# Seven block products in place of eight for the experts' first products, from group 5 on

## The reference, cut to what matters

```python
# attention with 32 packed rows per head; then, on x [2304, 512] (4 batches of 576 tokens):
def _moe_ref(x, w_gate, w1, w2):            # w1 [8, 512, 1024], w2 [8, 1024, 512]
    P = ...                                 # gates [2304, 8], 8 rounds of row and column scaling
    for e in range(8):
        h = np.maximum(x @ w1[e], 0.0)
        out += P[:, e:e + 1] * (h @ w2[e])
# then a two-layer MLP on the result (w_in [512, 2048], w_out [2048, 512])
```

## Time and profile before

| | |
|---|---|
| median of three runs | 1747.98 us |
| the profiled execution's own time | 1750.12 us |
| its span, first to last instruction | 1748.3 us |
| granted TensorE clock | 0.998 of full |
| PE busy | 1740.7 us (100%) |
| DVE / ACT / POOL busy | 909.5 / 709.8 / 608.7 us |
| mean DMA rate | 45 GB/s |

### The profile page before, as it was taken

The page is one execution under the profiler, slowest core; times in us unless marked ns, Lnnn a source line. Parts: engine busy times, 40 slices in busy tenths (PEclk is TensorE's granted clock), DMA queues, the critical chain, the costliest instruction groups (busy, mean ns, idle before and its releaser), DMA issues.

```text
span 1748.3 us, 27319 instructions
## 1 busy us (share of the span) xinstructions
PE 1740.7 (100%) x10257; PEld 1517.9 (87%) x10257; DVE 909.5 (52%) x1363; ACT 709.8 (41%) x1564; POOL 608.7 (35%) x380
## 2 busy tenths in 40 slices
PE   9999999999999999999999999999999999999999
PEld 7888888898889888988889888988888888888887
DVE  4846645444554454445444544454546555555545
ACT  4644465444434443444344443444343222222222
POOL 1254334444444344444444344444441001111100
PEclk9999999999999999999999999999999999999999
DMA  8431111111211111111211111112000000000002
GB/s 263 125 85 40 47 37 37 37 37 37 59 36 38 46 36 36 36 36 48 48 36 48 36 36 36 36 36 59 25 25 24 13 25 25 25 24 24 0 0 108
DMA packets 71776, 78.81 MB, mean 45 GB/s; under 512 B 7984, under 2 KB 59184, under 8 KB 71728
## 3 DMA queue, kind: packets, MB, share of 16 engines
q1 hardware_dynamic: 71728, 78.15, 16.6%
HBM read 73.42 MB, written 4.72 MB: 45 GB/s over the span
## 4 chain that ended last, share of the span: by engine, by line
PE 99%; ACT 0%; DMA 0%; SPq 0%; DVE 0%; issue 0%
PE PS L1223 96%; PE PS L1243 2%; PE PS L1457 0%; DMA k_raw<-k_dram 0%; ACT g_raw L621 0%; ACT acc L651 0%; PE PS L1427 0%; ACT acc L621 0%; SPq L441 0%; DVE stat L894 0%; DVE acc L1019 0%; SPq L422 0%; SPq L417 0%; ACT a_parts L621 0%; DVE stat L895 0%
## 5 line engine op out<-in xcount | busy, mean ns | idle before, releaser
L1223 PE MATMUL PS<-w_hi,h_hi 128*128 128x512 f32 x1440 | 562.9, 391 | 0.0
L1223 PE MATMUL PS<-w_hi,h_lo 128*128 128x512 f32 x1440 | 560.9, 390 | 0.0
L1223 PE MATMUL PS<-w_lo,h_hi 128*128 128x512 f32 x1440 | 560.7, 389 | 0.0
L1024 DVE SCALAR_TENSOR_TENSOR acc<-PS,gate,acc 128x512 f32<-128x512 f32 x504 | 378.0, 750 | 267.0 <-PE PS L1223 267.0
L698 ACT ACTIVATE h_hi<-PS 128x576 fp32r<-128x576 f32 x256 | 167.0, 653 | 671.6 <-PE PS L1223 670.9
L1223 PE MATMUL PS<-a_parts,g_parts 128*128 128x288 f32 x3072 | 438.2, 295 | 0.0
L1223 PEld LDWEIGHTS PS<-a_parts,g_parts 128*128 128x128 f32 x3072 | 419.4, 188 | 5.3 <-issue 0.4
L621 ACT ACTIVATE g_raw<-PS 32x256 f32<-32x256 f32 x992 | 372.8, 376 | 14.6 <-PE PS L1223 0.6
L1005 DVE SCALAR_TENSOR_TENSOR h_lo<-PS,h_hi 128x576 fp32r<-128x576 f32 x256 | 193.9, 757 | 324.1 <-ACT h_hi L698 324.0
L1223 PEld LDWEIGHTS PS<-w_hi,h_lo 128*128 128x128 f32 x1440 | 270.3, 188 | 57.1
L1223 PEld LDWEIGHTS PS<-w_hi,h_hi 128*128 128x128 f32 x1440 | 270.4, 188 | 54.4 <-DVE acc L1019 0.6
(11 more groups left out here) (130 smaller groups left out, 1046.9 us busy)
## 6 DMA issues: line engine op xcount, KB each, us to landing
stage<-moe_w_dram SPq DMA_DIRECT2D x96, 512.0 KB, 4.9
k_raw<-k_dram SPq DMA_DIRECT2D x8, 512.0 KB, 6.6
q_raw<-q_dram SPq DMA_DIRECT2D x8, 512.0 KB, 4.7
v_raw<-v_dram SPq DMA_DIRECT2D x8, 512.0 KB, 6.3
stage<-moe_w_in_dram SPq DMA_DIRECT2D x16, 256.0 KB, 2.8
stage<-moe_w_out_dram SPq DMA_DIRECT2D x8, 512.0 KB, 3.2
out_dram<-acc SPq DMA_DIRECT2D x16, 256.0 KB, 2.2
p_twice<-p_dram SPq DMA_DIRECT2D x8, 64.0 KB, 4.4
```

What stands on the lines that cost most here:

```text
L1024: return nc.vector.scalar_tensor_tensor(out=dst, in0=y, scalar=share, in1=dst, op0=ALU.mult, op1=ALU.add)
L1223: return nc.tensor.matmul(dst, lhsT, rhs, start=start, stop=stop)
```

## The change

From group 5 on (`SEVEN`), the first product of a batch, a 2 by 2 block matrix of G (128x128 blocks) by a 2 by 2 block matrix of A (128x288 blocks), is made of seven block products and fifteen sums of blocks (Winograd's form). Each product still takes three passes, so a batch takes 21 matmuls of 288 columns (`unit_of_seven` on PE). The sums stand on three engines:

- of A's blocks, once: POOL, in groups 1 to 4 (`sums_of_batch`, `first_sum_of_batch`), in `sums_of_a` and in place in `a_parts`;
- of G's blocks, in each group and batch: POOL (`blocks_of_batch`, eight instructions a batch), which takes the place of `split_products`;
- of the products: ACT copies the first out of its bank (`p1_copy`), DVE makes seven sums of 128x288 (`joins`): three into SBUF (`u2`, `u3`, `u4`), four back into the banks, where relu reads them.

The order of a group changes. It is now four pieces, each a unit (one batch) and then output tiles: batch 1 and tiles 0 to 4, batch 2 and tiles 5 to 8, batch 3 and tiles 9 to 13, batch 0 of the next group and tiles 14 to 17. The packed products (`fill`) stand behind the first tile of a piece, four matmuls each, and run up to two groups ahead; `g_raw` is there twice. In group 4 (`eight_to_seven`) the two forms meet. ACT's scaling of the second half of `acc` (`scale(1)`) moves from the middle of group 4 to its end.

```diff
+        BLOCKS = 7
+        G11, G22, G12, GS1, GS2, GS3, GS4 = range(BLOCKS)
...
+            def sums_of_batch(b):
+                cols = slice(b * S, (b + 1) * S)
+                a11, a12 = recombined[:, 0, 0:SPAN], recombined[:, 0, SPAN:S]
+                a21, a22 = recombined[:, 1, 0:SPAN], recombined[:, 1, SPAN:S]
+                t_link(nc.gpsimd.tensor_tensor(recombined[:], a_hi[:, :, cols].bitcast(F32),
+                                               a_lo[:, :, cols].bitcast(F32), ALU.add))
+                t_link(nc.gpsimd.tensor_tensor(a11, a12, a11, ALU.subtract))
+                t_link(nc.gpsimd.tensor_tensor(a12, a22, a12, ALU.subtract))
+                t_link(nc.gpsimd.tensor_tensor(a22, a22, a11, ALU.subtract))
+                t_link(nc.gpsimd.tensor_tensor(a21, a21, a22, ALU.subtract))
+                for t, full_sum in zip(sums_of_a, (a22, a12, a21)):
+                    t_link(nc.gpsimd.tensor_copy(t[:, 0, b, :], full_sum))
+                    t_link(nc.gpsimd.tensor_tensor(t[:, 1, b, :], full_sum, t[:, 0, b, :].bitcast(F32),
+                                                   ALU.subtract))
+
+            def first_sum_of_batch(b):
+                pool.wait_ge(h_full, hidden_count(SEVEN - 1, b, FC))
+                a11, a12 = (span[:] for span in spans_late)
+                first_span, second_span = slice(b * S, b * S + SPAN), slice(b * S + SPAN, (b + 1) * S)
+                for full_span, span in ((a11, first_span), (a12, second_span)):
+                    t_link(nc.gpsimd.tensor_tensor(full_span, a_hi[:, 0, span].bitcast(F32),
+                                                   a_lo[:, 0, span].bitcast(F32), ALU.add))
...
+            def blocks_of_batch(g, par, b):
...
+                wait_apart(pool, g_raw_ready, g * 4)
+                if isinstance(g, int) and g == SEVEN:
+                    pool.wait_ge(h_full, SEVEN * GC)
+                else:
+                    wait_apart(pool, seven_full, of_unit(g - 1, b, BLOCKS))
+                raw, hi, lo = raw_blocks(par, b), g_blocks[b][:, 0], g_blocks[b][:, 1]
+                g21, g11, g22, g12 = (raw[:, k, :] for k in range(4))
+                s1, s2, s3, s4 = (g_sums[:, k, :] for k in range(4))
+                nc.gpsimd.tensor_copy(hi[:, G11:GS1, :], raw[:, 1:4, :]).then_inc(g_step, 1)
+                nc.gpsimd.tensor_tensor(s1, g21, g22, ALU.add).then_inc(g_step, 1)
+                pool.wait_ge(g_step, step(2))
+                nc.gpsimd.tensor_tensor(s2, s1, g11, ALU.subtract).then_inc(g_step, 1)
+                pool.wait_ge(g_step, step(3))
+                nc.gpsimd.tensor_tensor(s4, g12, s2, ALU.subtract).then_inc(g_step, 1)
+                nc.gpsimd.tensor_tensor(s3, g11, g21, ALU.subtract).then_inc(g_step, 1)
+                wait_apart(pool, g_step, step(5))
+                nc.gpsimd.tensor_copy(hi[:, GS1:BLOCKS, :], g_sums[:]).then_inc(g_step, 1)
+                nc.gpsimd.tensor_tensor(lo[:, G11:GS1, :], raw[:, 1:4, :], hi[:, G11:GS1, :].bitcast(F32),
+                                        ALU.subtract).then_inc(g_step, 1)
+                pool.wait_ge(g_step, step(7))
+                nc.gpsimd.tensor_tensor(lo[:, GS1:BLOCKS, :], g_sums[:], hi[:, GS1:BLOCKS, :].bitcast(F32),
+                                        ALU.subtract).then_inc(g_split, 1)
+                wait_apart(pool, g_split, splits_until(g, b))
...
+            for g in range(1, SEVEN - 1):
+                sums_of_batch(g - 1)
+                ahead_of_group(g, g % 2, True)
+            sums_of_batch(B - 1)
+            first_sum_of_batch(0)
+            for Q in range(QUADS):
+                heads_after_fill(SEVEN + 1, Q)
+            first_sum_of_batch(1)
+            blocks_of_batch(SEVEN, 1, 0)
+            blocks_of_batch(SEVEN, 1, 1)
+            first_sum_of_batch(2)
+            first_sum_of_batch(3)
+            blocks_of_batch(SEVEN, 1, 2)
+            blocks_of_batch(SEVEN, 1, 3)
+
+            def group_of_seven(g, par):
+                ahead = MOE_GROUPS - 1 - g if isinstance(g, int) else 2
+                if ahead >= 2:
+                    heads_after_fill(g + 2, 0)
+                pool.wait_ge(y_full, g * TILES)
+                split_w2(g + 1, 1 - par)
+                if ahead:
+                    blocks_of_batch(g + 1, 1 - par, 0)
+                    blocks_of_batch(g + 1, 1 - par, 1)
+                    if ahead >= 2:
+                        heads_after_fill(g + 2, 1)
+                    else:
+                        pool.wait_ge(fill_full, fills_until(g + 1, 3))
+                        split_in(g + 2, par)
+                    blocks_of_batch(g + 1, 1 - par, 2)
+                    blocks_of_batch(g + 1, 1 - par, 3)
+
+            groups_of_seven(pool, group_of_seven)
...
+            def unit_of_seven(g, b):
+                act.wait_ge(seven_full, of_unit(g, b, P1))
+                copy(p1_copy, bank(C21B, SPAN)).then_inc(p1_copied, 1)
+                relu_joined(g, b, 1, C12)
+                relu_joined(g, b, 0, C21)
...
+            def group_of_seven(g, par):
+                ahead = MOE_GROUPS - 1 - g if isinstance(g, int) else 2
+                for n, (u, half, _, _) in enumerate(UNITS7):
+                    at = g + 1 if n == 3 else g
+                    if n < 3 or ahead:
+                        unit_of_seven(at, 2 * u + half)
+                    if n < 2 and ahead:
+                        shift_fill(g + 1, 1 - par, 2 + n)
+                    if n >= 2 and ahead >= 2:
+                        shift_fill(g + 2, par, n - 2)
...
+            scale(1)
+            unit_of_seven(SEVEN, 0)
+            for j in range(2):
+                shift_fill(SEVEN + 1, 0, j)
+            groups_of_seven(act, group_of_seven)
...
+            def joins(g, b):
+                dve.wait_ge(seven_full, of_unit(g, b, P6))
+                dve.wait_ge(p1_copied, units_until(g, b))
+                join(u2, C22B, p1_copy)
+                dve.wait_ge(seven_full, of_unit(g, b, P7))
+                dve.wait_ge(joined, of_unit(g, b, U2))
+                join(u3, C12B, u2)
+                dve.wait_ge(seven_full, of_unit(g, b, P2))
+                join(bank(C11B, SPAN), C11B, p1_copy)
+                dve.wait_ge(seven_full, of_unit(g, b, P5))
+                join(u4, C22B, u2)
+                dve.wait_ge(joined, of_unit(g, b, U3))
+                join(bank(C22B, SPAN), C22B, u3)
+                dve.wait_ge(seven_full, of_unit(g, b, P3))
+                dve.wait_ge(joined, of_unit(g, b, U4))
+                join(bank(C12B, SPAN), C12B, u4)
+                join(bank(C21B, SPAN), C21B, u3)
...
+            def unit_and_tiles(g, b, g_out, tiles, add, between=None):
+                joins(g, b)
+                for n, t in enumerate(tiles):
+                    output(g_out, t, add)
+                    if n < FC:
+                        lo_of_joined(g, b, 1 - n)
+                    if between:
+                        between(t)
...
+            def ahead_of_seven(g, u, t):
+                if u == 1 and t is not None:
+                    if t == 4:
+                        joins(SEVEN, 0)
...
+            def unit_of_seven(g, b):
...
+                pe.wait_ge(g_split, splits_until(g, b))
+                pe.wait_ge(h_lo_ready, hidden_count(g, b, 0))
+
+                def product(at_bank, block, tokens):
+                    three_passes([bank(at_bank, SPAN)], [g_blocks[b][:, part, block, :] for part in range(2)],
+                                 [tokens], True, True).then_inc(seven_full, 1)
+
+                product(C21B, G11, a11)
+                product(C22B, GS2, t2)
+                product(C12B, GS3, t3)
+                product(C11B, G12, a21)
+                pe.wait_ge(p1_copied, units_until(g, b))
+                product(C21B, G22, t4)
+                pe.wait_ge(joined, of_unit(g, b, U2))
+                product(C22B, GS1, t1)
+                pe.wait_ge(joined, of_unit(g, b, U3))
+                product(C12B, GS4, a22)
+
...
+            def fill(g, j):
+                Q, part = j // 2, j % 2
+                if part == 0:
+                    pe.wait_ge(w1_ready, g * 4 + (2 * Q + 2 - 4))
+                pe.wait_ge(g_raw_ready, g * 4 + (j - 5))
+                for hq in range(2):
+                    h, dst = 4 * Q + 2 * part + hq, bank(GB + part)[:, hq * FG:(hq + 1) * FG]
+                    mm(dst, pp_parts[:, h, :], by_head_hi[:, h, :], True, False)
+                    last = mm(dst, pp_parts[:, h, :], by_head_lo[:, h, :], False, True)
+                last.then_inc(fill_full, 1)
...
+            def group_of_seven(g, par):
+                ahead = MOE_GROUPS - 1 - g if isinstance(g, int) else 2
+                for n, (u, half, t0, t1) in enumerate(UNITS7):
+                    def behind(t):
+                        if t == t0 and n < 2 and ahead:
+                            fill(g + 1, 2 + n)
+                        if t == t0 and n >= 2 and ahead >= 2:
```

(17 more changed lines are left out.)

204 lines of the change are left out of this document (162 added, 42 removed).

## The result

The changed kernel takes 1734.18 us (median of four runs, 1731.23 to 1735.85), the kernel before 1747.96 beside it: a ratio of 0.992, interval 0.9903 to 0.9937. It is faster, by 13.8 us and not by the 40 forecast, and lies 6 us above the range. The profiled execution took 1731.23 us, with a span of 1729.4.

What follows compares the result with a forecast made beforehand. PE, busy throughout, was taken to bound the kernel: span 1748.3 - 43.1 (fewer matmuls) + 1.5 (meeting place) + 1.5 (met waits) = 1708.2 us. Forecast 1708.0, range 1704 to 1728, likeliest 1704 to 1714.

Steps and rivals of the forecast that it cites:

- the cover of the unit: DVE and ACT deliver joins and copy before PE's triples want them; PE passes each unit with about 0.4 us in hand.
- A: Rival: DVE's chain of joins and additions sets the piece, PE's fourth and fifth tiles come late; up to 1804 us; chance 0.14.
- the meeting place: Group 4 into 5, where old and new forms meet: PE waits for G's first batch; 1.5 us added (0 to 6).
- The PE term: Twelve fewer 288-column matmuls a group on PE, 1.60 us each group, 43.1 us over 27 groups; groups of 37.52 us.
- waits that are met: Five already met waits in each of 108 units on PE: 1.5 us added, between 0 and 6.
- C: Rival: met waits inside a unit break PE's matmul stream, up to 0.1 us each, up to 32 us: 1740; chance 0.09.
- my own line, that tiles keep 0.227 across a break: Evidence against C: output tiles have a wait and register instruction every six matmuls and keep 0.227 us.
- DVE's and ACT's ledger: Per group DVE has 32.3 us of 37.5, ACT 18.9, with joins at 0.455 us and ACT's copy at 0.40.
- the 1766 of A: Rival A's case with a pipe drain added to each join, 0.64 us a join: 1766 us.
- POOL: POOL feeds each group: batches of 5.9 us, a round of 34.0 of 37.5 us, waiting 3.5 us a round.

Runs made afterwards that it cites:

- The doubled body of the old kernel: The kernel before with VectorE's loop body doubled from four groups to eight, leaving one jump back: 1748.12 us (1.0003).
- 244: The changed kernel with VectorE's loop body cut to two groups, an inner loop of two iterations inside the loop over experts: 1711.8 us (0.9797).
- 268: The kernel before with ten increments of an unused semaphore on VectorE behind each group of its loop: 1747.56 us, one execution.
- 348: The kernel before with thirty increments of an unused semaphore on VectorE behind each group of its loop: 1760.17 us, one execution.
- the unrolled kernel: The changed kernel with VectorE's loop over experts 2 to 6 written out in full: 1711.71 us (0.9797 to the kernel before).
- four switches fewer: The changed kernel with VectorE's loop written out, and each unit's fill moved right behind its block products: 1709.27 us (0.9779).
- the hinted kernel: The changed kernel with a hint for the jump back on VectorE's loop over experts: 1715.44 us (0.9822).

## Why the prediction was wrong, and where it was right

**The step that failed** is the cover of the unit: "So PE passes the unit with about 0.4 us in hand". It was worked out for a unit whose joins DVE can issue when their inputs are there, and multiplied by 108. In four of them DVE has its loop's jump ahead of it, and stands for 3.95 us. I counted the change's work on DVE (28 joins a group) and not its instructions: they and their waits took the loop body from 228 to 468. The sum has no term for that, and none of the rivals holds it: A has DVE late in every piece, and would have shown 108 waits.

The second half of the same miss is that the place of the jump was safe before. The loop is old; what stood behind its jump then was an h_lo that DVE awaited for 1.5 us anyway. The change put in its stead a join that PE awaits. The doubled body of the old kernel shows the difference: a jump that stands for 2.85 us, of which PE feels 0.3.

The Trainium skill, "Runtime: NRT & Kernel Launch", section "Instruction fetch mechanics", has the rule: an engine's buffer holds two blocks, of 256 instructions each for an engine like DVE, is filled in order, and a taken branch to a target outside them stalls for a fetch. The runs agree in kind (no packet at the jumps for 228, 244, 268 and 348 instructions, packets for 454 and 468). They add that a body that fits by that size, 468 with a hint, is lost without one. That page of the Trainium skill gives no time for the stall; here it is 2.9 to 4.4 us in the chain of waits. The rule was open to me, and I didn't hold DVE's count of instructions against it; by its size alone, two blocks, it would have let 468 pass.

**The ledger of the miss**, from the span forecast to the one measured: 1708.2, + 18.9 for the four jumps (4.9, 3.7, 5.0, 5.3: by so much more each one puts PE's matmuls behind the same ones of the unrolled kernel), + 3.6 for groups of 37.71 us, - 0.2 at the meeting place, - 1.8 because the stretch before group 1 was so much shorter in this execution (the long unbroken pieces of PE's chain begin at 119.53, and at 121.34 before) = 1728.7, against 1729.4; 0.7 us are not assigned. This is the profiled execution, the fastest of the four. The other three took 2.2 to 4.6 us more, at a mean granted clock of 0.992 to 0.994 in place of 0.997; there is no trace of them, so where they lost it isn't shown.

**The PE term** was right in kind and a little large: groups take 37.71 us where I had 37.52. The 0.19 is 5.1 us in all, of which I had 1.5 for "waits that are met". Of it 0.08 went with four switches fewer; the distances of starts show it at tiles behind shorter matmuls (702.27, 702.51, 702.74 are 0.24 and 0.23 apart, where 0.227 is usual), and not within the units, which take the 2.77 us that they should (699.50 to 702.27; 21 x 0.133 is 2.79). So C was wrong in its place, and my own line, that tiles keep 0.227 across a break, was what hid it.

**DVE's and ACT's ledger** was right: 0.455 forecast and 0.456 to 0.458 measured, 0.40 and 0.412. One thing in it was too careful: joins that wait for nothing start 0.37 us apart, so three of them take 1.19 us and not 1.37, and the room is 1.0 us. With a drain added behind each, as the 1766 of A had it, they would start over 0.456 apart. The Trainium skill's section "The DRAIN you can't avoid" in "VectorE: DVE Perf Modes" has a sentence that A left out, "A next op that is not held starts earlier"; the trace agrees with it, and that of before had said so. A also has a slip: by its own rule, no change lies at a join of 0.61 to 0.62 us and not 0.62 to 0.63.

**POOL** came out at the forecast number: batches of 5.92 us (810.71 to 816.63), 3.34 us of waiting before batch 0 of a round where 3.5 was forecast. In part that is luck: the eight durations sum to 5.3 us where I had 5.8, and the gaps between them to 0.6 where I had 0.1:

```profile
810.71 0.51 POOL L719 CAST g_slots<-g_raw 128x384 fp32r<-128x384 f32 x1 [3.34 <-ACT g_raw L786]
811.18 0.46 POOL L720 TENSOR_TENSOR g_sums<-g_raw 128x128 f32<-128x128 f32 x1
...
814.98 1.29 POOL L731 TENSOR_TENSOR g_slots<-g_sums,g_slots 128x512 fp32r<-128x512 f32 x1
816.63 0.51 POOL L719 CAST g_slots<-g_raw 128x384 fp32r<-128x384 f32 x1 [0.36 <-POOL g_slots L731]
```

**The meeting place** had the right size (1.3 us against 1.5) for partly wrong reasons. The wait for the first batch of G is only 0.16 us; the rest is 0.56 for a late addition at 258.75 and 0.57 for ACT's first copy at 294.30. The wait for G:

```profile
282.62 0.67 PE L1497 MATMUL PS<-a_parts,g_slots 128*128 128x288 f32 x3 [0.16 <-POOL g_slots L731]
```

With the loop mended the kernel takes 1711.7 us, 3.7 above the forecast and inside its likeliest range. The arithmetic of the change held; what it did to the instruction stream wasn't in it.

## What to carry to other kernels

When a change adds work to an engine that runs a loop, count its instructions per iteration, waits and register instructions too, beside their time: look at the instruction queue's packets and for "issue" right behind the loop's line. Then ask what stands behind the jump back, and who waits for it. A smaller body, the loop written out, or a hint (which leaves one stall behind the loop) each took the stalls away here, where the body was the cause.

## What the runs showed of the hardware

- A jump back of DVE whose target isn't kept stands for 4.3 to 4.4 us in the changed kernel and for 2.85 in the old one with a doubled body. One packet of 8 KB (128 instructions) starts within it, one just after it. Bodies of up to 348 instructions are kept without a hint, 454 and more are not; in between isn't measured. With a hint 468 are kept, and DVE then idles 2.8 us once, 11 us behind the loop.
- After PE had idled for some 3.3 us, the granted clock stood at 1.2 GHz for a stretch in three of four cases; it cost 1.2 to 1.6 us each time beside the idle time itself. After 2.3 us, in the hinted kernel, its mean was 0.64 for 3 us.
- DVE instructions of 288 columns that wait for nothing start 0.36 to 0.38 us apart at a duration of 0.45 to 0.46.
- Matmuls of 512 columns right behind shorter ones start 0.23 to 0.24 us apart for some five of them, then 0.227.
